# The loaded rows of x in SBUF padded from 800 to 896 numbers

## The reference

```
w = exp(weight_gen - max); w = w / (sum(w) + 1e-9)             # over the 7 taps
x = sum over k of w[b, s, h, k] * x_pad[b, s + k, h, :]        # 7 positions, per head
h = x @ w_in                                                   # 192 -> 2048
P = a0 + a1*h + a2*h^2 + a3*h^3
Q = 1 + |b0|*|h| + |b1|*h^2
x = (P / (Q + 1e-6)) @ w_out                                   # 2048 -> 192
h = x @ w_in2
y = (h * clip(h + 3, 0, 6) / 6) @ w_out2
```

## Time and profile before

| | |
|---|---|
| median of three runs | 1311.78 us (1309.47 to 1312.77) |
| the profiled execution, its own time | 1315.33 us |
| its span, first to last instruction | 1313.5 us |
| instructions | 19407, among them 5128 matmuls |
| busy share PE / DVE / ACT / POOL | 93% / 92% / 91% / 83% |
| mean granted TensorE clock | 0.979 |

### The profile page before, as it was taken

How to read it: one execution, slowest core, us unless ns; L and a number is a source line. 1 busy time by engine, 2 the same in 40 slices (tenths; PEclk the granted TensorE clock), 3 DMA queues, 4 the chain that set the end, 5 groups by cost and what they waited for, 6 DMA issues and landing times.

```text
span 1313.5 us, 19407 instructions
## 1 busy us (share of the span) xinstructions
PE 1222.8 (93%) x5128; PEld 972.5 (74%) x5128; DVE 1208.1 (92%) x1898; ACT 1196.3 (91%) x2221; POOL 1093.7 (83%) x817
## 2 busy tenths in 40 slices
PE   2455999999999999999899999999999999999998
PEld 1344678887888778887688878887788888888876
DVE  5689999999999999999899999999999999999932
ACT  3878899999999999999799999999999999999954
POOL 5879889797998979798797979989797989965554
PEclk9679899999999999999899999999999999999999
DMA  5343222321312322230223213123222202000000
GB/s 169 94 117 77 68 60 55 79 49 42 77 39 60 74 60 48 60 74 27 59 56 78 49 44 76 38 60 74 60 49 60 66 29 49 13 17 2 13 12 13
DMA packets 61464, 73.62 MB, mean 56 GB/s; under 512 B 15912, under 2 KB 42280, under 8 KB 61096
## 3 DMA queue, kind: packets, MB, share of 16 engines
q1 hardware_dynamic: 61352, 72.35, 22.7%
HBM read 56.44 MB, written 8.01 MB: 49 GB/s over the span
## 4 chain that ended last, share of the span: by engine, by line
PE 67%; DVE 18%; issue 9%; ACT 5%; DMA 0%; POOL 0%; SPq 0%; POOLq 0%; ACTq 0%; DVEq 0%
PE h L653 7%; PE h L657 7%; PE h L655 7%; PE h L656 7%; PE h L654 7%; PE acc L661 7%; PE acc L663 6%; PE acc L662 6%; PE acc L665 6%; PE acc L664 6%; DVE early L1031 3%; DVE early L1025 3%; DVE early L1056 3%; DVE early L1019 3%; DVE q_recip L1040 2%
## 5 line engine op out<-in xcount | busy, mean ns | idle before, releaser
L592 POOL TENSOR_TENSOR g_lo<-early,g_hi 128x512 fp32r<-128x512 f32 x256 | 333.9, 1304 | 131.3 <-ACT g_hi L847 129.1
L601 POOL TENSOR_TENSOR g_lo<-late,g_hi 128x512 fp32r<-128x512 f32 x256 | 334.0, 1305 | 24.6 <-ACT g_hi L867 24.6
L653 PE MATMUL h<-x_hi,w_in_hi 128*128 128x512 f32 x512 | 209.8, 410 | 59.1 <-DVE early L1056 57.1
L1064 DVE SCALAR_TENSOR_TENSOR late<-late,h 128x512 f32<-128x512 f32 x256 | 174.8, 683 | 55.3 <-ACT late L858 54.3
L661 PE MATMUL acc<-g_hi,w_out 128*128 128x512 f32 x512 | 204.5, 399 | 5.4 <-DVE late L1076 3.0
L655 PE MATMUL h<-x_hi,w_in_lo 128*128 128x512 f32 x512 | 205.0, 400 | 0.0
L654 PE MATMUL h<-x_lo,w_in_hi 128*128 128x512 f32 x512 | 204.9, 400 | 0.0
L656 PE MATMUL h<-x_tail_hi,w_in_tail 128*128 128x512 f32 x512 | 204.8, 400 | 0.0
L657 PE MATMUL h<-x_tail_lo,w_in_tail 128*128 128x512 f32 x512 | 204.5, 399 | 0.0
L662 PE MATMUL acc<-g_hi,w_out 128*128 128x512 f32 x512 | 203.7, 398 | 0.0
L663 PE MATMUL acc<-g_lo,w_out 128*128 128x512 f32 x512 | 203.4, 397 | 0.0
(11 more groups left out here) (87 smaller groups left out, 2390.2 us busy)
## 6 DMA issues: line engine op xcount, KB each, us to landing
mix_w<-mix_weights SPq DMA_DIRECT2D x75, 192.0 KB
mix_w<-mix_weights SPq DMA_DIRECT2D x75, 144.0 KB
x_win<-in_x SPq DMA_DIRECT2D x15, 393.0 KB, 3.5
mix_w<-mix_weights SPq DMA_DIRECT2D x60, 96.0 KB
mix_w<-mix_weights SPq DMA_DIRECT2D x60, 72.0 KB
out_y<-late SPq DMA_DIRECT2D x16, 256.0 KB, 2.0
x_tail_hi<-tail_hi SPq DMA_DIRECT2D x60, 64.0 KB, 2.0
x_tail_lo<-tail_lo SPq DMA_DIRECT2D x60, 64.0 KB, 2.0
```

Source lines behind the costliest of these rows:

```text
L592: nc.gpsimd.tensor_tensor(g1_lo[p][:, :], neg_g[p], g1_hi[p][:, :].bitcast(F32), ALU.subtract).then_inc(g1_lo_ready, 1)
L601: nc.gpsimd.tensor_tensor(g2_lo[p][:, :], gate[p], g2_hi[p][:, :].bitcast(F32), ALU.subtract).then_inc(g2_lo_ready, 1)
L653: pe.matmul(out[:, :], w_hi[:, cols], hi[:, :], start=True, stop=False)
```

## The change

The constant `LINE` becomes 128 instead of 16. Nothing else uses it. The row of `x_win` grows from 16 x 50 = 800 numbers to 128 x 7 = 896 numbers; the kernel still uses 786 of them. All tensors made after it move up by 384 bytes in each partition.

```
 NB = TOKENS // BLOCK
 D2 = D - P
 SUB = P // H
-LINE = 16
+LINE = P
 WIN = HALF + HALO
 TPP = BLOCK // P
 PARTS = 8
```

## The result

The changed kernel takes 1293.74 us (median of four runs, 1292.41 to 1295.64), the kernel before, with a fourth run, 1311.77. The ratio is 0.9869, with a 95% interval of 0.9853 to 0.9885: 18.0 us or 1.3% faster. The faster rival came true, and by more than its price.

What follows compares the result with a forecast made beforehand. The prediction took TensorE's pace, the time between matmul starts, as the bound. All terms were taken as 0 us, giving no measurable difference and a median of 1311.8 us, with a range of 1296 to 1326 us.

Steps and rivals of the forecast that it cites:

- The faster rival: On PE, weight loads and matmul reads get out of each other's way: 3.1 ns less per matmul, 1297.5 us; chance 0.25.
- The bound: In the steady part TensorE sets the pace, busy 477.17 of 480 us, with VectorE 1.4% behind.
- the lever: Time between two matmul starts on PE, 0.2331 us; one ns per matmul is 4.6 us over the run.
- Addresses and instructions: Tensors after x_win shift 384 bytes, so moving tiles share the weights' remainder by 512; the same 19407 instructions, 0 us.
- its allowance: Seven ScalarE or VectorE instructions per chunk, each changed by 9 ns through operand addresses: 63 ns, hidden, taken as 0 us.
- 150 ns of cover: ScalarE's idle time per chunk of 4.69 us, said to hide longer instructions behind PE's pace.
- the open term: PE's price per matmul with moving tile and weights on one remainder: between 21.6 us less and 78 us more, taken as 0.
- two readings: On PE: three busy engines cost a matmul 0.3 ns, and steps ignore the weight slice's place; grounds for taking 0.
- The open term's lower bound: On PE the surplus over the columns' time vanishes: 0.2133 us per matmul, 92 us less before VectorE's limit.
- VectorE's cover of 94 ns per chunk: VectorE's idle time per chunk, said to allow a gain of 62 ns per chunk from shorter matmul steps.
- The bound of 21.6 us from VectorE: VectorE, busy 470.38 of 480 us, stops any gain from shorter matmul steps at 2.0% of 1080 us.
- The slower rival: On PE, both read streams start on one address class and meet more: 7 ns more per matmul, 1344 us; chance 0.21.

Runs made afterwards that it cites:

- e5: The kernel before with 128 bytes of padding ahead of each group of moving tiles, other tiles left 128 bytes off: 1292.45 us, ratio 0.9855.
- e4: TensorE alone, none of the kernel's work: 40 weight-load and matmul pairs for each of 72 slice placements; 226.7 ns per step at distance 0, 233.2 at 128 bytes.
- e7: The changed kernel with half of one VectorE product left out: 1284.22 us, ratio 0.9784; the kernel before with the same cut took 1302.03 us.
- e11: The changed kernel with half of a VectorE product and half of ScalarE's exponential left out: 1270.60 us; the kernel before with both cuts took 1298.15 us.
- e8: TensorE alone, none of the kernel's work, with weight columns, moving columns and number type varied: float32r 226.7 ns at distance 0, 233.5 at 128 bytes; bfloat16 215.8 at both.

## Why the prediction was wrong

*The bound was right.* The distance between matmul starts was the lever. The signs that the prediction gave for the faster rival all came: steps of 0.230 us or less, PE idle for more than 28 ns per chunk (43), and longer waits for L1056.

*Addresses and instructions were right*: 19407 instructions, the same products at 1.715 us, and no effect through other engines' tiles (e5). One count was off: ScalarE has eight instructions on 128x512 tiles per chunk (L814, L820, L826, L833, L839, L847, L858, L867, 256 of each in the run), not seven, so its allowance should have been 72 ns instead of 63; that is still under its 150 ns of cover.

*The step that failed is the one on PE, where I took 0 for the open term; the runs showed 5.84 ns less per matmul, 232.87 to 227.03.* The 0 had two readings behind it. The first, that three busy engines cost a matmul 0.3 ns, was sound and is confirmed by e4, which has the same steps, to within half a nanosecond, with TensorE alone. But it speaks of other engines' reads, not of TensorE's own two. The second, "the steps don't follow the weights' place", rested on slices 512 and 1536 bytes apart. Those are all multiples of 256, the period that e4 found. The trace of before held one single distance by 256 in 5120 pairs, so it couldn't tell "blind to the address" from "always at the same address". From this I drew "something inside PE that is blind to addresses", and that was the error. The prediction itself said further down that the rows don't prove it for the distance, and still gave it 0.54.

*The faster rival was right in kind and mis-sized.* Its term was 3.1 ns per matmul, measured 5.84. The open term's lower bound, where the surplus vanishes, was -20 ns; the chip stopped at 13 ns above the columns' time. VectorE's cover of 94 ns per chunk, which I held to be enough for 62 ns, became a limit with 117 (20 x 5.84): 77 ns per chunk came out. The bound of 21.6 us from VectorE held, at 18.0. But the limit is not VectorE's alone: e7 lowered VectorE's load and left the difference at 17.8 us, and only e11, with ScalarE lighter too, freed the rest.

*The slower rival* saw the effect in the right place, with the sign reversed: both streams start at the same moment on the same remainder, and that is the good case. Its price of +7 ns is close to what a distance of 128 costs above 0.

*The rule of the Trainium skill.* "TensorE: Matmul & The Clock Gate", section "Step-by-step: what each phase is for", says that loading the next weights takes no read bandwidth from the running matmul. For bfloat16 e8 agrees, with 215.8 ns at nine distances, close to the 215.7 that the page gives. For float32r the runs don't fit it as it stands: in e4 the step goes from 226.7 to 236.6 ns with nothing but the start of the moving slice changed, and stays at 226.7 when the weight slice moves along. Whether bandwidth is what is lost there, no run shows.

## What to carry to other kernels

Where float32r matmuls of 512 columns with 128 weight columns set the pace, look at the distance between the start of the moving tile and of the weight slice, modulo 256 bytes: 0 costs 226.7 ns per matmul, nearly all else 229 to 237 in e4. It costs only padding, but measure it for your own shape, since at 256 columns the best distance was 192 bytes and for bfloat16 it made no difference. How much of it arrives depends on the other engines: 18.0 us here, 27.6 us with two of them lighter. And before you call an effect absent in a trace, ask whether the trace has more than one value of the cause.

## What was not expected of the hardware

- The steps of float32r matmuls go through short cycles: at a distance of 0 they are 227, 227, 226 ns; at 128 bytes, 229 and 237 by turns, or seven steps of 228 to 241 ns. So two different cycles exist at the same distance, with means of 233.3 and 232.4 over whole cycles; the kernel before, with 232.87, shows steps of both.
- The step depends on starts as fine as 4 bytes: 226.7 ns at 28 bytes, 233.3 at 32, 236.6 at 4.
- With 256 moving columns a distance of 192 bytes takes 113.3 ns, 0 takes 120.0, 6% more.
- At distance 0 the surplus over the columns' time is 13.3 to 13.4 ns with 256, 384 and 512 moving columns alike; at 128 bytes it is 12.0, 15.9 and 20.2 ns (e8).
- What produces this inside TensorE stays open. Meetings of the two read streams fit that the distance counts and not the place; that fewer weight columns don't bring the surplus down towards nothing speaks against the simple form of it. Every set had a weight load ahead of each matmul, so what the step is without one wasn't measured.
